# A three-stage kernel's attention stage, rearranged: heads on 128 partitions with nine tokens each, products on quarters of the array, tokens in strip order

## The reference, cut to what matters

```python
# q, k, v: (8 batches, 8 heads, 576 tokens, 64); all float32
kv  = einsum('bhsd,bhse->bhde', k, v)            # 64 x 64 for each head
out = einsum('bhsd,bhde->bhse', q, kv)
rms = sqrt(mean(out * out, axis=-1) + 1e-6)
x   = out / rms * g_norm                         # then (4608 tokens, 512)
x   = (sigmoid(x @ w_gate) * (x @ w_val)) @ w_out    # 512 -> 1536 -> 512
h   = x @ w_in                                   # 512 -> 2048
y   = where(h > 0, h, exp(min(h, 0)) - 1) @ w_out2   # 2048 -> 512
```

## Time and profile before

| | us |
|---|---|
| three runs | 1681.03, 1682.70, 1689.64 |
| median | 1682.7 |
| the profiled execution | 1679.23 |
| its span | 1677.2 |

### The profile page before, as it was taken

The page is one execution under the profiler, slowest core; times in us unless marked ns, Lnnn a source line. Parts: engine busy times, 40 slices in busy tenths (PEclk is TensorE's granted clock), DMA queues, the critical chain, the costliest instruction groups (busy, mean ns, idle before and its releaser), DMA issues.

```text
span 1677.2 us, 26049 instructions
## 1 busy us (share of the span) xinstructions
PE 1627.0 (97%) x9912; PEld 1558.7 (93%) x9912; DVE 1233.7 (74%) x1501; ACT 832.6 (50%) x1251; POOL 180.3 (11%) x185
## 2 busy tenths in 40 slices
PE   7989999999999999999999999999999899999999
PEld 5778899999999999999999999999999788888888
DVE  5778888886588754777777666676774788888886
ACT  6656555565455544444444544544553444444443
POOL 6564222220022100000000000000000000000000
PEclk9999999999999999999999999999999899999999
DMA  9994488878788545554444664324429744433332
GB/s 278 278 306 150 160 305 315 315 295 313 255 308 307 200 164 215 202 218 148 151 151 151 225 264 144 140 104 142 142 104 343 271 134 154 147 131 127 126 130 81
DMA packets 194738, 339.23 MB, mean 202 GB/s; under 512 B 13376, under 2 KB 149568, under 8 KB 194624
## 3 DMA queue, kind: packets, MB, share of 16 engines
q1 hardware_dynamic: 194624, 337.69, 57.6%
HBM read 191.89 MB, written 145.75 MB: 201 GB/s over the span
## 4 chain that ended last, share of the span: by engine, by line
PE 74%; DVE 7%; ACT 5%; issue 4%; DMA 2%; POOL 0%; SPq 0%; ACTq 0%; DVEq 0%; POOLq 0%
PE pair L927 37%; PE pair L960 16%; PE pair L991 13%; PE pair L993 7%; DVE e L1589 2%; DMA u_elu<-e 2%; DVE s L1460 1%; ACT e L1244 1%; ACT e L1284 1%; ACT e L1279 1%; ACT ring L1110 1%; DVE s2b L1460 1%; DVE s5b L1460 1%; DMA u_elu<-s 1%; ACT s L1267 0%
## 5 line engine op out<-in xcount | busy, mean ns | idle before, releaser
L927 PE MATMUL pair<-ring,wreg 128*128 128x384 f32 x5040 | 886.5, 336 | 17.0 <-ACT s L1267 6.9
L927 PEld LDWEIGHTS pair<-ring,wreg 128*128 128x128 f32 x5040 | 878.0, 189 | 24.6 <-ACT s L1267 10.4
L991 PE MATMUL pair<-wreg,ring 128*128 128x512 f32 x1008 | 351.6, 393 | 3.1 <-ACT s L1303 3.0
L1460 DVE TENSOR_TENSOR s<-s,pair 128x768 f32<-128x768 f32 (+1 forms) x216 | 190.8, 883 | 142.6 <-PE pair L927 111.3
L993 PE MATMUL pair<-wreg,ring 128*128 128x256 f32 x1008 | 282.9, 281 | 0.0
L960 PE MATMUL pair<-ring,wreg 128*128 128x384 f32 x1512 | 262.2, 334 | 0.0
L960 PEld LDWEIGHTS pair<-ring,wreg 128*128 128x128 f32 x1512 | 262.1, 188 | 0.0
L991 PEld LDWEIGHTS pair<-wreg,ring 128*128 128x128 f32 x1008 | 189.2, 188 | 45.6 <-ACT s L1303 3.4
L1384 DVE TENSOR_TENSOR ring<-raw,ring 128x1024 fp32r<-128x1024 f32 (+1 forms) x162 | 180.6, 1133 | 68.2 <-ACT ring L1120 53.2
L993 PEld LDWEIGHTS pair<-wreg,ring 128*128 128x128 f32 x1008 | 191.2, 190 | 0.0
L1244 ACT ACTIVATE e<-e 128x768 f32<-128x768 f32 x72 | 61.0, 847 | 191.2 <-DVE e L1589 191.2
(11 more groups left out here) (112 smaller groups left out, 1604.9 us busy)
## 6 DMA issues: line engine op xcount, KB each, us to landing
wreg<-weight_items SPq DMA_DIRECT2D x98, 512.0 KB, 6.3
raw<-u_elu SPq DMA_DIRECT2D x36, 1024.0 KB, 7.3
u_gated<-ub SPq DMA_DIRECT2D x144, 192.0 KB, 2.7
weight_items<-out_w SPq DMA_DIRECT2D x50, 512.0 KB, 4.6
weight_items<-out_x SPq DMA_DIRECT2D x48, 512.0 KB, 4.6
x_raw<-x_attention SPq DMA_DIRECT2D x48, 384.0 KB, 5.3
raw_k<-u_gated SPq DMA_DIRECT2D x6, 2304.0 KB, 8.3
raw<-u_gated SPq DMA_DIRECT2D x12, 1152.0 KB, 5.7
```

The costliest lines, as they stand in the source:

```text
L927: mm = pe.matmul(dst[:, g, 0:NT], w[:, a, cols], ring[:, slot, b, kt, :], start=(i in STARTS and kt == a == b == 0), stop=(kt == 1 and a = ...
L991: pe.matmul(dst[:, 0, :], s[:, 0, 2 * c + kt, :], w[:, :, cols], start=(i in STARTS and c == kt == 0), stop=False, skip_group_check=True)
L1460: dve.tensor_tensor(acc, acc, pp, ALU.add).then_inc(s_comb, 1)
```

## The change

A head pair is loaded as 128 partitions: each head has 64 partitions with nine tokens each (2304 B in a row, where there were 1536). A "strip" t is the tokens 9r + t of a head, r from 0 to 63. There is no q copy. Two neighbouring strips of both heads are transposed in one step of 128 x 128, five steps for the pairs of strips 0, 2, 4, 6 and 7 (of the last one only strip 8 is used). The transposed even strips stand in rows 0 to 63 and the odd ones in rows 64 to 127, for either head.

KV is formed in nine steps of 64 tokens for each head, head 0 on the array's first row half and first column half into pair1, head 1 on the second of both into pair3, which is the bank of RB[0]. Since even and odd strips need KV on their own rows, each head's KV is copied twice: head 0 by DVE, head 1 by ACT. kv·qt is four products of 64 rows by 64 columns: 256 tokens (four even strips) for the two heads, then 320 tokens (five odd ones). All that follows works on parts of 256 and 320 tokens instead of two of 288, and tokens stay in strip order in x and in all later stages; the last store writes each half of 64 rows to rows 9 apart of the result, so it is two DMAs.

K·V of pair p now also waits for the first norm of lap p−1 (it frees the bank), and the r product of a lap waits for ACT's copies of KV. The square sums stand ahead of the r product. All loops are written out. The seven splits of weight chunk 1 stand behind laps 6 to 17, and the four loads of x behind laps 18, 20, 22 and 24 instead of together behind lap 24.

```diff
-    SP_ = 96
-    RT = S // SP_
+    HALF_ = 64
+    RT = S // HALF_
+    EVEN, ODD = (RT - 1) // 2 * HALF_, (RT + 1) // 2 * HALF_
...
-    CHUNK_UNIT = {1: 0, 2: 1, 3: 3, 4: 4, 5: 6, 6: 7, 7: 9, 8: 10, 9: 12, 10: 13, 11: 15,
+    CHUNK_UNIT = {2: 1, 3: 3, 4: 4, 5: 6, 6: 7, 7: 9, 8: 10, 9: 12, 10: 13, 11: 15,
...
-        KV, MS = pair[1][:, 0, :], pair[1][:, 1, :]
+        MS = pair[1][:, 1, :]
+        KV = (pair[1][0:D, 0, 0:D], pair[3][D:P, 0, EVEN:EVEN + D])
...
+        STRIP_PAIRS = (0, 2, 4, 6, 7)
+        STRIPS = (0, 2, 4, 6, 1, 3, 5, 7, 8)
+        WIDTH = (EVEN, ODD)
...
+            X_PIECE = {18: 0, 20: 1, 22: 2, 24: 3}
...
@@ store of the result @@
-                row = (2 * (n - FIRST4) + th) * TT
-                sp.dma_start(out[row:row + TT, 256 * fh:256 * fh + 256], src[:, 0, :]).then_inc(
-                    s_st[NAMES.index(c)], 16)
+                for m in range(2):
+                    batch, strip = divmod((2 * (n - FIRST4) + th) * 2 + m, RT)
+                    rows = out[batch * S:(batch + 1) * S, 256 * fh:256 * fh + 256].rearrange("(r t) f -> t r f", t=RT)
+                    sp.dma_start(rows[STRIPS[strip]], src[m * HALF_:(m + 1) * HALF_, 0, :]).then_inc(
+                        s_st[NAMES.index(c)], 16)
...
@@ PE, a lap @@
+                    for m, t in enumerate(STRIP_PAIRS):
+                        bank, at = divmod(m, 4)
+                        if at == 0:
+                            wait_count(pe, s_qt_sb, 2 * p + bank - 1)
+                        mm = pe.transpose(QT[bank][:, at * P:(at + 1) * P],
+                                          qkv[:, slot, 0, t:t + 2, :].rearrange("r t d -> r (t d)"), ident[:, :])
...
+                    for h in range(2):
+                        wait_count(pe, s_kv_sb[h], 2 * p)
+                    if valid(p - 1, LB):
+                        pe.wait_ge(s_x, 2 * (p - 1 - LB) + 1)
                     for t in range(RT):
                         for h in range(2):
                             rows = slice(h * D, (h + 1) * D)
-                            mm = pe.matmul(KV[rows, rows], qkv[:, r % QR, 1, h, t, :], qkv[:, r % QR, 2, h, t, :],
+                            mm = pe.matmul(KV[h], qkv[rows, slot, 1, t, :], qkv[rows, slot, 2, t, :],
                                            start=(t == 0), stop=(t == RT - 1))
...
-                        pe.matmul(O[c][:, 0:HN], kv[:, (r - LO) % 2, :], qt[:, (r - LO) % 2, half(c)],
-                                  start=True, stop=True).then_inc(s_o_ps, 1)
+                        rows = slice(c * D, (c + 1) * D)
+                        for h in range(2):
+                            strips = qt[rows, n % 2, 0:WIDTH[c] // D, h, :]
+                            mm = pe.matmul(O[c][h * D:(h + 1) * D, 0:WIDTH[c]], kv[rows, n % 2, h, :], strips,
+                                           start=True, stop=True)
+                        mm.then_inc(s_o_ps, 1)
...
                     pe.wait_ge(s_rlo, n // NP + 1)
+                    if valid(p, 0):
+                        pe.wait_ge(s_kv_sb[1], 2 * p + 2)
...
@@ ACT, a lap @@
+                if valid(p, 0):
+                    act.wait_ge(s_kv_ps, p + 1)
+                    for c in range(2):
+                        act.activation(kv[c * D:(c + 1) * D, p % 2, 1, :], KV[1], ACT.Copy).then_inc(s_kv_sb[1], 1)
...
@@ DVE, a lap @@
-                if ahead:
-                    copy_q(trip, r + LC)
...
+            EARLY = {0: (0, P6), 1: (0, P5), 2: (0, P7), 3: (0, P3), 4: (0, P4), 6: (1, P1), 7: (1, P2), 9: (1, P6),
+                     11: (1, P5), 13: (1, P7), 15: (1, P3), 17: (1, P4)}
+            for p in range(PAIRS + LB):
+                step(p)
+                if p in EARLY:
+                    split_weight(*EARLY[p])
```

More of the change, by code:

```diff
@@ L48, in build @@
     QR = 4
[L49 to L50 removed]
+    assert S == HALF_ * RT and RT == 9 and D == HALF_ and (T, DM, F1, F2) == (4608, 512, 1536, 2048)
     ITEMS = 7
@@ L469, in load_chunk, with step @@
+            def step(p):
+                if 1 <= p <= PAIRS - QR:
+                    sp.wait_ge(s_kv_ps, p)
+                    load_pair(p + QR - 1)
+                if valid(p, LB):
+                    n = p - LB
+                    hp = n % NP
+                    sp.wait_ge(s_x, 2 * n + 2)
+                    sp.dma_start(x1_dram[hp * P:(hp + 1) * P, n // NP * S:(n // NP + 1) * S],
+                                 o[:, n % RING, :]).then_inc(s_xst[n % RING], 16)
             def load_chunk(c):
@@ new lines, in step @@
+                        mm.then_inc(s_o_ps, 1)
+                if valid(p, LM):
+                    n = p - LM
+                    m = n % NP
+                    if n == 0:
+                        pe.wait_ge(s_cast, 2)
+                    if m == 0:
+                        wait_count(pe, s_rms, n // NP)
+                    for c in (1, 0):
+                        pe.wait_ge(s_sqhi, 2 * n + c + 1)
+                        first = factor_rows(n, c) * P
+                        w = sum_w[:, :, :].rearrange("p n c -> p (n c)")[:, first:first + P]
+                        pe.matmul(MS[:, 0:WIDTH[c]], w, sq_hi[:, n % 2, c, 0:WIDTH[c]],
+                                  start=(m == 0 and c == 1), stop=False)
+                        pe.wait_ge(s_sqlo[c], n + 1)
+                        mm = pe.matmul(MS[:, 0:WIDTH[c]], w, sq_lo[:, n % 2, c, 0:WIDTH[c]], start=False,
+                                       stop=(m == NP - 1 and c == 0))
+                    mm.then_inc(s_ms, 1)
@@ L893, in _ @@
-            static_steps(step, 0, RING)
-            looped_steps(pe, step, 1, TRIPS)
+                        w = spread_w[:, factor_rows(n, c)].rearrange("p h d -> p (h d)")
+                        b2 = n // NP % 2
+                        pe.matmul(RB[c][:, 0:WIDTH[c]], w, r_hi[:, b2, 0:WIDTH[c]], start=True, stop=False)
+                        pe.matmul(RB[c][:, 0:WIDTH[c]], w, r_lo[:, b2, 0:WIDTH[c]], start=False, stop=True).then_inc(
+                            s_rb, 1)
+            for p in range(PAIRS):
+                step(p)
@@ L1004, in _ @@
             gated_product(0, P6)
-            static_steps(step, PAIRS + 3, PAIRS + 5)
-            pe.wait_ge(s_kv_sb, 2 * PAIRS)
+            for p in (PAIRS + 3, PAIRS + 4):
+                step(p)
+            for h in range(2):
+                pe.wait_ge(s_kv_sb[h], 2 * PAIRS)
             pe.wait_ge(s_rms, B)
             gated_product(0, P5)
-            static_steps(step, PAIRS + 5, PAIRS + LB)
+            for p in (PAIRS + 5, PAIRS + 6):
+                step(p)
             for i in range(P7, ITEMS):
@@ L1650, in out_unit @@
                         sum_u2(vis + 1, name)
-            for r in range(LC):
-                copy_q(0, r)
             dve.wait_ge(s_const, CONSTANTS)
```

312 lines of the change are left out of this document (121 added, 191 removed).

## The result

| | before | changed |
|---|---|---|
| median of 6 and 6 runs, us | 1682.76 | 1696.45 |
| lowest and highest | 1681.03, 1689.64 | 1693.59, 1699.11 |
| the profiled execution | 1679.23 | 1699.11 |

The medians differ by 13.7 us; the ratio is 1.0073 [1.0048, 1.0098], 12 us (8 to 16) slower. Both are more than the 8.4 us from which a change can be told here, though the lower end of the interval is not. So the forecast "no change, 1685" had the sign of its sum right and its size too small by 11.6.

The account below looks back on a forecast made before the run. The prediction took the PE's own order of work to bound attention; +10.8 − 1.4 − 1.6 − 6.0 + 0.3 = +2.1 us, against the median of 1682.7 a forecast of 1685 us, range 1669 to 1700.

Parts of the forecast that it names:

- no change, 1685: Whole kernel: the forecast's own case, two large terms that cancel to +2.1 us, within 1677 to 1691; chance 0.45.
- the clock rival: Attention batch ends: waits at K·V lower the clock, about 1.6 us each, 9.6 in all, 1695; chance 0.18.
- Attention laps 9 to 32: Attention: K·V's new wait makes laps of 4.45 us, 1.55 more at six batch ends; 111.7 against 100.9, +10.8 us.
- If only the PE's own lap counted (3.7), 94.4: Attention, lower bound of the laps' term: PE's own lap of 3.7 us with Q·KV's quarters overlapping wholly, −6.5 us.
- the ring: Attention: one-lap chain from K·V through Q·KV, o, squares, sq_lo and norm to the next K·V, 4.45 us.
- The x tiles: Late attention: loads spread over laps end the DVE's wait and K·V's 4.76 us wait; already counted in the 111.7.
- First pairs, −1.4: Start of attention, 9 to 41 us: first transpose some 0.9 us earlier without the q copy; bounds 0 and −4.
- End of attention, −1.6: Last K·V: its 1.93 us wait and the slower products behind it go; −1.6 us, bounds 0 and −3.
- Units, −6.0: Units 0 and 1: moving chunk 1's splits out of unit 0 removes PE waits and slow products; bounds −1 and −7.
- Output stage, +0.3: Output stage: a store becomes two, SP idles, so only the last one counts; bounds 0 and +1 us.
- The queues were the bound: Attention, faster rival: DMA queues bound it and loads have fewer descriptors; 1670, chance 0.27 together with a short ring.
- Quarters don't overlap: Attention, slower rival: 64-row products do not run side by side, lap 5.3 us, 20 us more, 1705; chance 0.10.

Follow-up runs that it names:

- second profile: The changed kernel itself, run and profiled once more with nothing altered: median 1696.25 us, 1.0068 to the kernel before.
- the ring open: Changed kernel with the two norms of a lap ahead of the low squares, alone or with one more edit: 23 laps 92.3, 90.6 and 88.2 us.
- before, split stores: The kernel before with each output quarter stored by two DMAs of 64 rows instead of one: 1687.02 us, ratio 1.0014.
- the norm first: The changed kernel with the two norms of a lap ahead of the low squares in the DVE's order: 1672.25 us, ratio 0.9922.

## Why the prediction was right or wrong

The measured 1696 lies in the stated range of 1669 to 1700, but the forecast's own case, no change at 1685, did not come. The mechanism of its largest term was right; what it missed are the terms around it: 2.9 us ahead of the laps, 2.4 behind them, 4.5 in the units and 3.2 in the output stage, against 1.5 that the laps were shorter. That 1696 stands next to the clock rival's 1695 is luck: in the second profile the clock's falls cost the 23 laps nothing. Of the prediction's own signs, laps of 4.3 to 4.6 us and waits for "DVE o" came, and no gap above 1 us in units 0 and 1 did not (1.50).

- **Attention laps 9 to 32: right.** 4.40 us a lap for 4.45, 1.50 at a batch's end for 1.55. Link by link, predicted and measured: K·V to Q·KV 1.20, 0.96; Q·KV to o 0.80, 0.83; to the squares 0.46, 0.47; to sq_lo 0.63, 0.70; to the norm 0.84, 0.82; to the next K·V 0.52, 0.62. That the whole lap holds to 0.05 is partly luck: the first step was 0.24 shorter than forecast and the others together 0.19 longer. The term was 9.3 without falls of the clock, and 12.6 in the first profile, with three (2.6 us for two batch ends, 0.7 for the ninth lap).
- **"If only the PE's own lap counted (3.7), 94.4": mis-sized.** The PE's own lap is 3.54: K·V to Q·KV 0.96, Q·KV to the sums 0.78, the eight products 1.17, transposes 0.63. A K·V record takes 0.030 us (33 from 60.86 to 61.85), and it took as long before: the last two of the 24 start at 58.62, 0.69 behind the first. So the prediction's 0.024 was a wrong reading, and its 0.26 between K·V and Q·KV was 0.15, from the start of the last K·V record to Q·KV. That is what is gone: Q·KV now starts ahead of the last three K·V records, and half as many records again add 0.12 us to the step and not 0.36. With the ring open the 23 laps were 92.3, 90.6 and 88.2, under the bound. The kernel before, the end of K·V and the start of Q·KV:

```profile
58.62 0.23 PE L856 MATMUL pair<-qkv 96*64 96x64 f32 x2
58.77 0.51 PE L865 MATMUL pair<-qt,kv 128*128 128x288 f32 x1
```

- **The x tiles:** gone, as said, but mostly for another reason, the longer laps; the spacing took a last wait of 1.11 us on the DVE.
- **First pairs, −1.4: failed.** I counted the loads and not the wait; the ring starts at the ninth pair, whose K·V stands 6.45 us behind the eighth one's in both profiles and 4.4 in the two kernels with the ring open. There the ninth K·V starts at 38.8 and 39.2, −2.2 and −1.9: the term was right for a kernel without the ring. The second profile's +1.5 also holds a later first K·V (11.65 instead of 9.99).
- **End of attention, −1.6: failed.** The last lap waits 1.33 us at K·V, ahead of it 0.80 at the r product, and runs at half clock (1.96 us) as before. I had the wait of the batch's end in the ring and left it out here.
- **Units, −6.0: failed in size, −1.5 in the second profile.** The moved splits are worth 4.3 to 5.2; 2.8 us come in from elsewhere, of which the waits of later units, which I did not have, are 1.8, and 1.50 us of the gap stays. The term also counted 3.1 us of slow products that the kernel before does not have in every execution (none in "before, split stores").
- **Output stage, +0.3: mis-sized, 3.5 us in the second profile, 2.4 by the ratios.** "SP idles, so only the last one counts" looked at the issue. The last one alone costs 0.9. What else counts is the landing: the store of quarter 12 stands behind a 2 MB load, and its quarter's next snapshot waits for it. It was late in no unit of the kernel before, in 4 with whole stores in the changed kernel, and in 5 to 10 of 18 with split stores behind the load.
- **The rivals.** The clock did fall at batch ends, at 8 of 30 in the five profiles whose attention is the changed kernel's (3, 2, 1, 1 and 1 of six), 1.3 us each where the lap counts among the 23 (1.6 forecast). The prediction had the rival decide once the wait at K·V nears 2 us; waits of 1.24 to 1.33 did it at 7 of 29, and the one of 1.96 did. So the mechanism is real, and not reliable enough to be the forecast. "The queues were the bound" fell: from the ninth pair on every wait at K·V was for the norm, with the DMA engines 0.78 busy. "Quarters don't overlap" fell: 33 records in 0.99 us, where the prediction's 0.048 one by one makes 1.58. The Trainium skill (TensorE: Matmul & The Clock Gate, Part 3: Packing small matmuls) has them at work at once, and the trace agrees with these 0.99 us. The Trainium skill's rule that a change of the tiling mode drains the engine (TensorEngine Tiling (Array Packing), Key Properties) fits too: 0.15 us lay between the last K·V record and Q·KV in different modes, none in the same one. No run tells the drain from another cause.

## What to carry to other kernels

When a buffer is shared by two steps of one loop, follow the new wait backwards through the *order* of the engine that releases it. Here the release stood behind an unrelated operation that depended on the same lap, and this made a ring of one lap; two lines in another order took 24 us off the same kernel. The split store was late by its place behind a 2 MB load and not by its issue: look for who reuses a store's source, and what large load stands ahead of it. And a single profile of a kernel that runs for 1.7 ms can differ from the next by more than the effect in question, here by the clock's falls and by the pitch of a unit; compare stretch by stretch, with a second profile.

## What the runs showed of the hardware

- The output stage's products ran at 0.347 or 0.353 us a pair of records in different executions of one program and in different units of one execution, with the granted clock at 1.00 in both (19.41 and 19.79 us a unit). The stages ahead did not move with it (633.5 to 634.7 us from the middle stage to the output stage in all). What it is stays open.
- K·V's 64-row, 64-column products from two quarters follow at 0.030 us a record, into two banks or into one; the 96-row products of the kernel before, on two column halves, at the same pace.
- sq_lo of 256 columns takes 0.87 to 0.96 us on the DVE where POOL squares for some 0.6 us beside it, and 0.42 in the plain laps with the norm first, where POOL has squared already and its own subtraction runs beside it (1.08 us there, 0.87 otherwise).
- A wait of 1.24 to 1.33 us at K·V, 0.80 before it, was followed by half clock at 7 of 29 batch ends, and not at the same ones in two executions of one program.
